# Hash bits in four products a head: high and low projection side by side, both column halves in one bank

## The reference

```python
q_bits = (np.einsum('bhsd,dk->bhsk', q, proj) > 0)        # proj: 64 x 6
k_bits = (np.einsum('bhsd,dk->bhsk', k, proj) > 0)
q_bucket = np.sum(q_bits * 2 ** np.arange(6), axis=-1)     # the same for k
mask = q_bucket[:, :, :, None] == k_bucket[:, :, None, :]
scores = np.where(mask, scale * (q @ k.T), -1e9)
attn = softmax(scores);  out = attn @ v
```

## Time and profile before

| | us |
|---|---|
| median of 3 runs (lowest, highest) | 718.14 (718.07, 718.44) |
| profiled execution | 718.99 |
| its span, first to last instruction | 717.2 |
| TensorE busy | 707.4 (99%) |
| VectorE, ScalarE, GpSimd busy | 405.7, 342.7, 329.2 |
| mean granted TensorE clock | 0.995 |

### The profile page before, as it was taken

One profiled execution on the slowest core, in us unless ns is written; L12 is line 12 of the kernel. 1 busy time (PEld: TensorE's weight loads), 2 busy tenths in 40 slices (PEclk: granted clock), 3 DMA queues, 4 the chain that ended last, 5 costly groups with the idle time before them and its releaser, 6 DMA issues.

```text
span 717.2 us, 10761 instructions
## 1 busy us (share of the span) xinstructions
PE 707.4 (99%) x3746; PEld 606.0 (84%) x3746; DVE 405.7 (57%) x828; ACT 342.7 (48%) x694; POOL 329.2 (46%) x295
## 2 busy tenths in 40 slices
PE   7999999999999999999999999999999999999998
PEld 5899999999999897888888888888888888888876
DVE  5998998999999568432221121212424467744443
ACT  4999999999999665233111111111232433222111
POOL 5688888889979779553000000110053655211100
PEclk8999999999999999999999999999999999999999
DMA  6354555445432123220000001010012110000002
GB/s 183 95 137 109 138 135 144 107 122 142 115 90 79 31 59 117 73 90 30 0 1 1 0 1 45 31 50 0 1 46 87 45 67 15 4 27 16 16 30 88
DMA packets 39508, 45.97 MB, mean 64 GB/s; under 512 B 15546, under 2 KB 26936, under 8 KB 39456
## 3 DMA queue, kind: packets, MB, share of 16 engines
q1 hardware_dynamic: 36016, 41.16, 20.3%
q0 software_dynamic: 3296, 4.09, 2.4%
q10 hardware_dynamic: 144, 0.05, 0.0%
HBM read 29.23 MB, written 3.15 MB: 45 GB/s over the span
## 4 chain that ended last, share of the span: by engine, by line
PE 90%; DVE 6%; issue 1%; POOL 1%; ACT 1%; DMA 0%; DVEq 0%; POOLq 0%; ACTq 0%
PE PS L1035 21%; PE PS L1037 21%; PE PS L1036 21%; PE PS L1128 7%; PE PS L1173 4%; PE PS L1172 4%; PE PS L1191 4%; PE PS L1192 4%; DVE negmax L1422 1%; DVE ETL L1431 1%; PE PS L1283 1%; PE PS L1139 1%; PE PS L1208 1%; DMA const<-in_projb_dram 0%; DVE X L1399 0%
## 5 line engine op out<-in xcount | busy, mean ns | idle before, releaser
L1580 DVE SCALAR_TENSOR_TENSOR HL<-PS,HH 128x512 fp32r<-128x512 f32 x48 | 33.2, 691 | 154.3 <-ACT HH L1021 154.3
L1021 ACT ACTIVATE HH<-PS 128x512 fp32r<-128x512 f32 x48 | 28.7, 598 | 183.4 <-PE PS L1037 183.4
L903 ACT ACTIVATE E<-PS,bias,factor 128x768 f32<-128x768 f32 x96 | 95.5, 994 | 13.9 <-DVE factor L1425 7.7
L1422 DVE TENSOR_REDUCE negmax<-PS 128x1 f32<-128x768 f32 x96 | 91.0, 948 | 13.1 <-PE PS L1173 13.0
L1431 DVE TENSOR_TENSOR ETL<-PS,ETH 128x384 fp32r<-128x384 f32 x192 | 97.2, 547 | 1.3 <-ACT ETH L896 1.2
L896 ACT ACTIVATE ETH<-PS 128x384 fp32r<-128x384 f32 x192 | 83.4, 488 | 2.1 <-PE PS L1128 0.5
L1128 PE MATMUL PS<-ident,E 128*128 128x128 f32 x576 | 79.8, 274 | 0.1
L1035 PE MATMUL PS<-UTH,W 128*128 128x512 f32 x192 | 75.7, 394 | 0.0
L1035 PE MATMUL PS<-W2H,HH 128*128 128x512 f32 x192 | 74.8, 390 | 0.2 <-DVE HL L1580 0.2
L1037 PE MATMUL PS<-UTH,W 128*128 128x512 f32 x192 | 74.8, 390 | 0.0
L1037 PE MATMUL PS<-W2H,HL 128*128 128x512 f32 x192 | 74.7, 389 | 0.0
(11 more groups left out here) (205 smaller groups left out, 1553.8 us busy)
## 6 DMA issues: line engine op xcount, KB each, us to landing
RAW<-in_moe_w_ch_dram SPq DMA_DIRECT2D x32, 256.0 KB, 2.7
QK<-in_qk_dram SPq DMA_DIRECT2D x16, 384.0 KB, 4.3
VR<-in_v_dram SPq DMA_DIRECT2D x16, 192.0 KB, 2.7
out_dram<-fin SPq DMA_DIRECT2D x12, 256.0 KB, 2.0
QM<-TOPH SPq DMA_DIRECT2D x15, 192.0 KB, 2.8
KM<-TOPL SPq DMA_DIRECT2D x15, 192.0 KB, 3.1
TOPL<-QM SPq DMA_DIRECT2D x15, 192.0 KB, 2.7
TOPH<-TOPH SPq DMA_DIRECT2D x15, 192.0 KB, 3.0
```

Source lines behind the costliest of these rows:

```text
L903: nc.scalar.activation(E[:, tile % NE, :], s_bank(tile)[:, 0:S], ACT.Exp, bias=bias[:, t:t + 1], scale=factor[:, t:t + 1], accum_out=esum[ ...
L1422: nc.vector.tensor_reduce(negmax[:, t:t + 1], s_bank(tile)[:, 0:S], AX_X, ALU.max, negate=True).then_inc(s_max, 1)
```

## The change

For heads 2 to 15 one bits unit a head remains, in slot 5 two heads ahead, with four products for six. PJ holds two sets of weights of 120 columns, one for each column half: columns 0 to 55 the high projection, columns 64 to 119 the low one, and within each 56 the 24 columns in use begin at 0 in set 0 and at 32 in set 1; the rest is zero. TOPH goes through all 120 columns, TOPL through the first 56. So rows 0 to 23 of the bank hold half 0, rows 32 to 55 half 1 (high x high and high x low together), and rows 64 to 119 the low projection's part of the same. ScalarE copies 120 x 384 to MB. SyncE moves rows 64 to 119 to BL (`move_bits`), GpSimd adds BL to rows 0 to 55 and then makes the mask rows, MR being 56 x 384 now. Four DMAs of 12 x 384 for two of 12 x 768 take it to QM and KM. Head 1 keeps six products, now in one unit in slot 0. The core of the diff:

```diff
-            units.append(("bits", h + 1, 1))
...
             def move_in(h):
-                sp.wait_ge(s_ring, done["bits", h, 1])
+                sp.wait_ge(s_ring, done["bits", h, 0])
...
+            def move_bits(h):
+                sp.wait_ge(emptied["bits"], h)
+                sp.dma_start(BL[:], MB[ML:MP]).then_inc(s_bl, 16)
...
-                sp.dma_start(QM[D:D + NM, b].bitcast(F32), MR[0:NM].bitcast(F32)).then_inc(s_mask, 16)
-                sp.dma_start(KM[D:D + NM, b].bitcast(F32), MR[KROW:MW].bitcast(F32)).then_inc(s_mask, 16)
+                for i in range(2):
+                    c, row = slice(i * HC, (i + 1) * HC), i * KROW
+                    sp.dma_start(QM[D:D + NM, b, c].bitcast(F32), MR[row:row + NM].bitcast(F32)).then_inc(s_mask, 16)
+                    sp.dma_start(KM[D:D + NM, b, c].bitcast(F32), MR[row + NM:row + 2 * NM].bitcast(F32)).then_inc(s_mask, 16)
...
                 move_in(h)
+                if h > 1:
+                    move_bits(h)
                 move_mask(h)
...
+            pool.memset(PJ[:].bitcast(F32), 0.0).then_inc(s_init, 1)
...
             def mask_rows(h):
-                pool.wait_ge(emptied["bits"], 2 * h)
-                pool.wait_ge(s_mask, 32 * (h - 1))
-                nc.gpsimd.tensor_scalar(MR[:], MB[:], gamma[:, 0:1], gamma[:, 1:2], ALU.is_gt, ALU.mult).then_inc(s_mr, 1)
+                pool.wait_ge(s_bl, 16 * (h - 1))
+                nc.gpsimd.tensor_tensor(MB[0:MC], MB[0:MC], BL[:], ALU.add).then_inc(s_mb, 1)
+                pool.wait_ge(s_mb, h - 1)
+                pool.wait_ge(s_mask, 64 * (h - 1))
+                nc.gpsimd.tensor_scalar(MR[:], MB[0:MC], paired[:, 0:1], paired[:, 1:2], ALU.is_gt, ALU.mult).then_inc(s_mr, 1)
...
-                    last = product(bank[0:MW, 0:HC], projH[:], TOPH[:, h % 3, c], projL[:], TOPL[:, h % 3, c], True, True)
+                    if h == 1:
+                        pe.wait_ge(s_proj, 5)
+                        for c in range(2):
+                            last = product(bank[0:MC, 0:HC], PJ[:, c, 0:MC], TOPH[:, h % 3, halved[c]], PJ[:, c, ML:MP],
+                                           TOPL[:, h % 3, halved[c]], c == 0, c == 1)
+                    else:
+                        nc.tensor.matmul(bank[0:MP, 0:HC], PJ[:, 0, :], TOPH[:, h % 3, halved[0]], start=True, stop=False)
+                        for c in range(2):
+                            nc.tensor.matmul(bank[0:MC, 0:HC], PJ[:, c, 0:MC], TOPL[:, h % 3, halved[c]], start=False, stop=False)
+                        last = nc.tensor.matmul(bank[0:MP, 0:HC], PJ[:, 1, :], TOPH[:, h % 3, halved[1]], start=False, stop=True)
```

More of the change, by code:

```diff
@@ L26 @@
 MW = KROW + NM
+MC = KROW + 2 * NM
+ML = 2 * KROW
+MP = ML + MC
 SCALE = D ** -0.5
@@ L125, in program @@
     einv = put("einv", [P, NSTAT])
[L126 to L129, removed]
+    const = put("const", [P, 2 * MW + 4])
+    proj2 = put("proj2", [P, 2 * KROW])
+    PJ = put("PJ", [P, 2, MP], F32R)
     gamma = const[0:MW, 2 * MW:2 * MW + 2]
+    paired = const[0:MC, 2 * MW + 2:2 * MW + 4]
     stats = put("stats", [P, NT, 6])
@@ L145, in program @@
     region = used[0]
-    MB = put("MB", [MW, S], F32, un_at)
+    MB = put("MB", [MP, HC], F32, un_at)
+    BL = put("BL", [MC, HC])
     src_at = tail - 4 * 2 * DM
@@ L288, in turned_pair, with columns_of, part_of @@
             return ap.rearrange("p (a b) -> p b a", b=HALF)
+        def columns_of(tile):
+            return tile[:].rearrange("p (a b) -> p a b", b=KROW)[:, :, 0:NM]
+        def part_of(tile, i, at):
+            return tile[:, i, at + i * KROW:at + i * KROW + 2 * NM].rearrange("p (a b) -> p a b", b=NM)
         def blocks(ap):
@@ L346, in program @@
         s_mr = sem("s_mr")
+        s_bl = sem("s_bl")
+        s_mb = sem("s_mb")
         s_away = sem("s_away")
@@ L717, in _ @@
             turned = E[:, NE - 1, :]
-            pool.wait_ge(s_init, 4)
+            pool.wait_ge(s_init, 5)
             pool.wait_ge(s_const, 16)
-            nc.gpsimd.tensor_tensor(proj2[:], const[:, 0:MW], const[:, MW:2 * MW], ALU.mult).then_inc(s_proj, 1)
+            nc.gpsimd.tensor_tensor(proj2[:, 0:MW], const[:, 0:MW], const[:, MW:2 * MW], ALU.mult).then_inc(s_proj, 1)
             pool.wait_ge(s_proj, 1)
-            nc.gpsimd.tensor_copy(projH[:], proj2[:]).then_inc(s_proj, 1)
-            pool.wait_ge(s_proj, 2)
+            for i in range(2):
+                nc.gpsimd.tensor_copy(part_of(PJ, i, 0), columns_of(proj2)).then_inc(s_proj, 1)
             pool.wait_ge(s_turned, 16)
@@ L728, in _ @@
             pool.wait_ge(s_first_key, 2)
-            nc.gpsimd.tensor_tensor(projL[:], proj2[:], projH[:].bitcast(F32), ALU.subtract).then_inc(s_proj, 1)
-            pool.wait_ge(s_proj, 3)
+            for i in range(2):
+                pool.wait_ge(s_proj, 2 + i)
+                nc.gpsimd.tensor_tensor(part_of(PJ, i, ML), columns_of(proj2), part_of(PJ, i, 0).bitcast(F32), ALU.subtract).then_inc(s_proj, 1)
             pool.wait_ge(s_top, 2)
@@ L922, in _ @@
                             act.wait_ge(s_mr, h - 2)
-                        nc.scalar.activation(MB[:, c], ring(unit_no[u])[0:MW, 0:HC], ACT.Copy).then_inc(emptied["bits"], 1)
+                        nc.scalar.activation(MB[:], ring(unit_no[u])[0:MP, 0:HC], ACT.Copy).then_inc(emptied["bits"], 1)
                     elif kind == "back":
@@ L1129, in unit @@
                 elif kind == "bits":
-                    c = slice(i * HC, (i + 1) * HC)
+                    halved = [slice(c * HC, (c + 1) * HC) for c in range(2)]
                     pe.wait_ge(s_top, 2 * h)
-                    if h == 1 and i == 0:
-                        pe.wait_ge(s_proj, 3)
-                    last = product(bank[0:MW, 0:HC], projH[:], TOPH[:, h % 3, c], projL[:], TOPL[:, h % 3, c], True, True)
+                    if h == 1:
[8 more added lines that the diff above has]
+                        last = nc.tensor.matmul(bank[0:MP, 0:HC], PJ[:, 1, :], TOPH[:, h % 3, halved[1]], start=False, stop=True)
                 elif kind == "back":
@@ L1641, in mask_constants @@
     signs = np.concatenate([np.repeat([1, -1], BITS), np.zeros(KROW - NM), np.repeat([-1, 1], BITS)])
-    gamma = np.zeros((P, 2))
-    gamma[0:MW] = [[0, 1]] * BITS + [[-TINY, 1]] * BITS + [[0, 0]] * (KROW - NM) + [[-TINY, -PEN]] * BITS + [[0, -PEN]] * BITS
+    gamma = np.zeros((P, 4))
+    gamma[0:MW, 0:2] = [[0, 1]] * BITS + [[-TINY, 1]] * BITS + [[0, 0]] * (KROW - NM) + [[-TINY, -PEN]] * BITS + [[0, -PEN]] * BITS
+    for i in range(2):
+        gamma[i * KROW:i * KROW + NM, 2:4] = gamma[0:NM, 0:2]
+        gamma[i * KROW + NM:i * KROW + 2 * NM, 2:4] = gamma[KROW:MW, 0:2]
     return np.concatenate([np.tile(signs, (P, 1)), gamma], axis=1).astype(np.float32)
```

17 lines of the change are left out of this document (7 added, 10 removed).

## The result

The changed kernel takes 749.07 us (median of 4 runs, 746.65 to 749.64), the kernel before 718.11 beside it: a ratio of 1.0424, 95% interval 1.0406 to 1.0441. The forecast was 723.0 with a range of 715 to 729. The sign and the closed loop of the forecast were right, the size was not: 31 us were lost where 4.8 were forecast. Nor does TensorE gain by itself, as the forecast had it. The profiled execution is the fastest of the four, 746.65 us (span 744.9, granted clock 0.993).

A forecast was written before the change was run, and what follows sets the result against it. TensorE bounds the kernel before at 14.12 us a head; after the change a 14.55 us loop through SyncE's queue binds from head 3, a loss of 4.8 us on 718.99, less 0.85 to the median: 723.0 us, range 715 to 729.

The forecast's parts named there:

- closed loop of the forecast: Once a head, SyncE's moves, their landing, move_bits, GpSimd, mask DMAs and V's load wait in a circle: 14.55 us.
- What bounds the kernel: TensorE, busy 99% of the span, bounds the kernel before at 14.12 us a head; SyncE's queue had slack.
- so no wait is added there: Bits unit on TensorE: the ring of three banks is used by one unit less, so no added wait.
- 13.77: TensorE's head period in us after the change: 14.12 less 0.52 in slot 1 plus 0.17 in slot 5.
- rival 1: The loop doesn't bind, being under 13.77 us; all of TensorE's saving is kept, 713.4 us; chance 0.15.
- The start: Head 1's six products delay tile 1's scores by 0.96 us, mostly made up again; loss taken as 0.2 us.
- The round trip: GpSimd must await move_bits in SyncE's queue; the loop needs 14.55 us a head, TensorE 13.77; loss 4.8 us in all.
- 3.53: Loop term in us: move_away's second issue to landing, 0.64 and 0.59 for issues plus the 2.3 wait at L527.
- in a closed loop they always do, so 2.3: Wait at L527: the moves always follow V's load directly, so 2.3 us and not 1.8.
- 14.55: Length in us of one loop through SyncE's queue and GpSimd with no idle in it, the sum of eight terms.
- The short issues: Mask DMA issues of 12 rows stay dear with half the columns, 3.28 us for four; move_bits' 56 rows dear too.
- Rival 3: move_bits lands late, 3.2 us, behind QK's load and move_in; loop 15.05 us, 729 us in all; chance 0.08.

The follow-up runs named there:

- no_low: The changed kernel without move_bits and without GpSimd's add, so the low projection's part of the bits is left out: 725.36 us, ratio 1.0112.
- act_evict: The changed kernel without move_bits; ScalarE copies the bank in two pieces and shifts the low rows to partitions 0 to 55 itself: 726.65 us, ratio 1.0149.
- tables_first: The changed kernel with GpSimd's 14 table loads issued in heads 1 to 3 (five, five, four), not one a head: 746.67 us, ratio 1.0399.
- before_four: The kernel before with each of its two mask DMAs cut in two by columns, four of 12 x 384: 720.7 us, ratio 1.0046.
- before_fold: The kernel before with GpSimd's five pieces of fold work moved from slot 5 to behind the mask rows in slot 2: 718.53 us, ratio 1.0013.
- tables_late: The changed kernel with each of GpSimd's 14 table loads issued behind its head's mask rows (slot 2), not at slot 0: 738.68 us, ratio 1.0282.
- act_os_edge: act_os with VectorE's small fold of an edge row one slot earlier in head 14: 717.64 us, ratio 0.9991.
- act_os: act_evict with ScalarE's copy of OT to OS ahead of that slot's exponential instead of behind it: 723.01 us, ratio 1.007.

## Why the prediction was wrong

**What bounds the kernel: right.** TensorE led, and what had to be looked for was in SyncE's queue.

**TensorE: one step failed.** Slot 1 lost 0.52 and slot 5 gained 0.19 for 0.17. But "so no wait is added there" is wrong: I looked at the ring of three banks, in which the unit lay, and not at the bank OT, whose copy the unit had hidden by standing ahead of the products. Slot 2 pays 0.44, so that TensorE's own head is 14.25 and not 13.77, for 14.10 before, and the change was a loss on TensorE by itself. So rival 1 had no room: with the loop open the ratio is still 1.011 to 1.015 (no_low, act_evict, some 3 us of it head 14's stall). In the changed kernel this is hidden under the longer loop.

**The start: not settled.** I took 0.2. The changed kernel's head 2 starts at 36.19 and other kernels with its beginning start it at 36.3 to 38.9 (tables_first, with its table loads there, left out); the kernel before starts it at 37.22, and before_four and before_fold, with the same beginning, at 36.56 and 34.58. The executions differ by more than the term.

**The round trip: right in mechanism, wrong in one term.** It binds, with its stations, the waits and V's load followed by the next move in 0.62 to 0.65 us as said. move_bits takes 2.8 us to the add in most heads against 2.7. Four mask DMAs take 3.10 for 3.28. The failed term is "3.53", from move_away's second issue to its landing; with the 0.58 ahead of it it was 4.11 and measured 5.59. I took the 2.3 us wait at L527 from the heads of the earlier trace rows in which the moves follow V's load, and said "in a closed loop they always do, so 2.3". In those rows the table load came 1.8 to 2.3 us after move_away. In the closed loop it comes 0.3 to 1.8 us before it in heads 2 to 9, 1.1 in most of them, and 0.1 to 0.9 after it in the others: GpSimd's work and SyncE's now wait for each other, and a load issued ahead of GpSimd's work for a head lies just where the moves are. The loads did not change; their phase did. The term is 19 of the 23.7 us by which the loops exceed 14.55 x 13. How much of it is the loads and how much their place, two kernels tell: without loads the mean term is 4.28 (tables_first, from head 5 on), so about 17 of the 19 go with the loads; with the same loads 3.8 to 5.2 us ahead of move_away it is 4.48 (tables_late), so about 14 go with their place, though the kernel's time fell by 10 only. Without a load near, the term was 4.0 to 4.5, about as forecast.

The kernel before had one such landing, which the two waits of the earlier trace rows leave out: in head 7 the 579 KB load of SSH is issued 1.06 us after move_away, and this row of its DMAs from 91.5 to 99.5 us has 4.7 where the median is 3.1.

```profile
KM<-TOPL SPq DMA_DIRECT2D x1, 192.0 KB, 4.7
```

**The rest of the loop.** Where nothing of the tables is left (tables_first from head 5 on) a loop is still 15.21: 0.17 in the first term, 0.20 from move_in to move_bits, 0.19 from there to the add, where GpSimd comes late in some heads, and 0.09 in the others. These I have read from traces and not tested one by one.

**The short issues: right.** Measured 0.71 to 0.79 us for 12 rows, whatever the columns; move_bits' issue is 0.83 for 56 rows, where 64 rows take 0.46 to 0.60 in the loop shown. By the rule of the Trainium skill that the forecast weighed (DMA: Bandwidth & Descriptors, section Why a DMA increments its semaphore by 16 and not by 1) 56 rows go on 14 engines and the issuing sequencer writes the missing two counts. That this makes an issue dear was the forecast's inference, and the 0.83 us agree with it for 56 rows as well.

**The rivals.** Rival 3, a move_bits that lands late and 729 us, named the right kind of fault at the wrong transfer: move_away was the late one, and by 1.5 us a loop in the mean, not 0.5.

## What to carry to other kernels

Before a piece of work is taken from a full engine, look for the waits that it hides, on every buffer that its neighbours use and not only on its own. Before a DMA is put into a queue, add up each round trip that passes through that queue; once it binds, everything that was timed by the old rhythm shifts against it, and a background load of another queue can land on the transfer that the loop waits for, so price a landing with that load beside it. A shift between partitions costs 0.5 us when it is made by the engine that empties the bank, and here took the place of a DMA with 2.8 us of latency; it turned a kernel that was 4.2% slower into one that, with three small moves (OT's copy and the two folds), is 0.2% faster.

## What the runs showed of the hardware

**A small VectorE instruction can take as long as GpSimd's.** FX<-X, one row of 255 numbers, takes 0.40 us (act_os_edge above). In no_low, VectorE and GpSimd from 214 to 219 us:

```profile
215.38 3.20 DVE L1388 TENSOR_TENSOR FX<-X 1x255 f32<-1x255 f32 x1
...
214.86 1.64 POOL L625 TENSOR_SCALAR MR<-MB,const 56x384 fp32r<-56x384 f32 x1
216.49 1.80 POOL L657 TENSOR_TENSOR FE<-AE 128x765 f32<-128x765 f32 x1
```

It started within the first of GpSimd's two and ended 0.29 us after the second, as the two-number copy of act_os ended with its pair. With a single GpSimd instruction beside it, einv took 0.67 us for 0.16 (before_fold above). VectorE's instructions that read PSUM ran beside GpSimd at their usual length: in the kernel before, beside the 2.93 us of mask rows from 142.45, the row maximum took 0.95 us and a pair of L1431 1.01.

The Trainium skill knows this as an exclusive lock on a port pair that VectorE and GpSimd share (SBUF — State Buffer, section Who interferes with whom): whoever comes first has it for its whole instruction, and a VectorE instruction with two inputs from SBUF, or a copy in its two-port mode, needs it. The 3.20 for 0.40 us agree; that VectorE is not let in between two GpSimd instructions that follow each other, so that the wait is for both, is what these traces show beyond it.

**ScalarE shifts rows as it empties a bank.** Its copy of rows 64 to 119 of a PSUM bank to partitions 0 to 55 of BL costs what the unshifted one does. ScalarE in act_evict:

```profile
124.54 0.47 ACT L944 ACTIVATE MB<-PS 56x384 f32<-56x384 f32 x1
125.03 0.49 ACT L945 ACTIVATE BL<-PS 56x384 f32<-56x384 f32 x1
```
